# Decay attention, soft MoE and GELU layer on one core: the order of work in a pair of heads changed, one score product instead of two, and the first expert's w1 loaded last

## What is computed

```python
for t in range(S):                      # _attn_ref, r k v w: [4, 8, 768, 48]
    cur = einsum('bhd,bhe->bhde', u * kt, vt)
    y[:, :, t] = einsum('bhd,bhde->bhe', rt, state + cur)
    state = wt[..., None] * state + einsum('bhd,bhe->bhde', kt, vt)
logits = x @ phi                        # _moe_ref, x: [3072, 384]
d = softmax(logits, 0); slot_input = d.T @ x
slot_out[e] = relu(slot_input[e] @ w1[e]) @ w2[e]
x = softmax(logits, 1) @ slot_out
h = x @ w_in                            # _moe2_ref
out = (h * sigmoid(1.702 * h)) @ w_out
```

## Time and profile before

| what | value |
|---|---|
| profiled execution | 416.04 us |
| its span, first to last instruction | 414.1 us |
| TensorE busy | 400.3 us, 97% of the span |
| VectorE, ScalarE, GpSimd busy | 250.2, 186.8, 49.0 us |
| granted TensorE clock, mean | 1.000 |
| DMA | 69.00 MB, mean 167 GB/s |

### The profile page before, as it was taken

The page is one execution under the profiler, slowest core; times in us unless marked ns, Lnnn a source line. Parts: engine busy times, 40 slices in busy tenths (PEclk is TensorE's granted clock), DMA queues, the critical chain, the costliest instruction groups (busy, mean ns, idle before and its releaser), DMA issues.

```text
span 414.1 us, 9544 instructions
## 1 busy us (share of the span) xinstructions
PE 400.3 (97%) x3723; PEld 315.3 (76%) x3723; DVE 250.2 (60%) x463; ACT 186.8 (45%) x412; POOL 49.0 (12%) x50
## 2 busy tenths in 40 slices
PE   7989999999999879999999999999999999999996
PEld 5868787887888633545888888888888888888885
DVE  5878877987888574515767445454544545454542
ACT  5667777786787411504443422422242242224221
POOL 3432342233422200000000000000000000000000
PEclk9999999999999999999999999999999999999999
DMA  7999999899899398993000200010010001001001
GB/s 260 405 357 342 350 351 335 298 351 350 298 343 356 140 408 354 368 406 126 1 0 2 78 0 0 9 67 2 0 76 0 0 9 69 0 2 76 2 0 76
DMA packets 15589, 69.00 MB, mean 167 GB/s; under 512 B 1600, under 2 KB 1728, under 8 KB 14528
## 3 DMA queue, kind: packets, MB, share of 16 engines
q1 hardware_dynamic: 15552, 68.47, 44.0%
HBM read 63.75 MB, written 4.72 MB: 165 GB/s over the span
## 4 chain that ended last, share of the span: by engine, by line
PE 87%; DVE 5%; DMA 3%; ACT 3%; issue 2%; DVEq 0%; SPq 0%; ACTq 0%
PE bank L1022 31%; PE bank L1026 16%; PE bank L996 5%; PE bank L761 5%; PE bank L856 4%; PE bank L833 4%; PE bank L923 3%; PE bank L957 3%; PE bank L848 3%; DMA rk<-rk_in 2%; PE bank L767 2%; PE bank L799 2%; PE bank L814 2%; PE bank L790 2%; PE bank L774 1%
## 5 line engine op out<-in xcount | busy, mean ns | idle before, releaser
L522 ACT ACTIVATE ring<-bank 128x512 f32<-128x512 f32 x96 | 57.4, 598 | 139.4 <-PE bank L996 139.3
L728 DVE CAST g_hi<-ring 128x512 fp32r<-128x512 f32 x96 | 40.8, 425 | 88.8 <-ACT ring L522 88.8
L1022 PE MATMUL bank<-g_hi,wo_hi 128*128 128x512 f32 x285 | 80.1, 389 | 0.0
L1022 PE MATMUL bank<-g_hi,wo_lo 128*128 128x512 f32 x285 | 80.0, 389 | 0.0
L1026 PE MATMUL bank<-g_lo,wo_hi 128*128 128x512 f32 x285 | 80.0, 389 | 0.0
L730 DVE TENSOR_TENSOR g_lo<-ring,g_hi 128x512 fp32r<-128x512 f32 x96 | 66.5, 693 | 3.3
L1022 PEld LDWEIGHTS bank<-g_hi,wo_hi 128*128 128x128 f32 x285 | 53.4, 188 | 11.2 <-DVE g_hi L728 0.2
L1022 PEld LDWEIGHTS bank<-g_hi,wo_lo 128*128 128x128 f32 x285 | 53.5, 188 | 11.1
L1026 PEld LDWEIGHTS bank<-g_lo,wo_hi 128*128 128x128 f32 x285 | 53.5, 188 | 11.1
L996 PE MATMUL bank<-cst,mst 128*128 (+1 forms) x96 | 37.4, 391 | 0.1
L596 DVE TENSOR_TENSOR at<-bank,causal 128x512 f32<-128x512 f32 x48 | 30.1, 683 | 12.0 <-PE bank L833 11.7
(11 more groups left out here) (137 smaller groups left out, 440.7 us busy)
## 6 DMA issues: line engine op xcount, KB each, us to landing
nat<-nat_in SPq DMA_DIRECT2D x32, 576.0 KB, 6.0
rk<-rk_in SPq DMA_DIRECT2D x16, 768.0 KB, 7.0
ring<-w_in SPq DMA_DIRECT2D x16, 768.0 KB, 7.8
w2a<-w_in SPq DMA_DIRECT2D x4, 1536.0 KB, 12.4
out_t<-ring SPq DMA_DIRECT2D x5, 768.0 KB, 3.5
ring<-w_in SPq DMA_DIRECT2D x2, 1536.0 KB, 8.3
ring<-win_in SPq DMA_DIRECT2D x4, 768.0 KB, 10.2
ring<-wout_in SPq DMA_DIRECT2D x4, 768.0 KB, 15.0
```

The costliest lines, as they stand in the source:

```text
L522: a.activation(gact[:, s % NG, :], bank[6 + s % 2][:, :], ACT.Gelu_apprx_sigmoid).then_inc(g_done, 1)
L728: v.tensor_copy(g_hi[:, s % NG, :], gact[:, s % NG, :]).then_inc(ghi_done, 1)
L1022: t.matmul(bank[3 * par + o][:, :], wo[:, f, P * o:P * (o + 1)], g_hi[:, s % NG, :], start=(f == 0 and wo is wo_hi), stop=False)
```

## The change

- log_sums of the next pair stands whole (twelve records, one semaphore step) behind the scores; before, half of it stood ahead of them. exps waits for the whole, and makes both inverses first, then both exponentials.
- A score unit is one product of 128 keys against 128 tokens; the memsets of banks 2 to 4 go, with the wait for them.
- The x transposes of both halves stand together behind both halves of the value products; ScalarE evacuates both y halves first, then both x tiles.
- The logarithm is taken one pair ahead instead of two, ahead of scaled_states; w is rolled by one pair, and only w of pair 0 is loaded on its own.
- VectorE does the bonus of a pair ahead of front of the next pair. GpSimd's first product of each pair waits for front (f_done) of that pair.
- Both halves of w1 of expert 0 are loaded behind the loop instead of ahead of it.

```diff
@@ sync
-            sp.dma_start(w01[:, 0, :], w01_in[0]).then_inc(ld_w[0], 16)
+            sp.dma_start(w0, w0_in).then_inc(ld_w, 16)
             load_rk(0, 0)
-            sp.dma_start(w01[:, 1, :], w01_in[1]).then_inc(ld_w[1], 16)
...
-            load_w1(0, 0)
-            load_w1(0, 1)
             with sp.Fori(1, PAIRS // 2) as m:
...
+            for q in range(2):
+                load_w1(0, q)
             sp.dma_start(w2_early[:, :], w2_in[NE - 1]).then_inc(ld_w2[NE - 1], 16)
@@ gpsimd, pair
                 if s.first:
                     pool.wait_ge(ld_u, 16)
-                    pool.wait_ge(f_done, 1)
+                pool.wait_ge(f_done, s.i + 1)
@@ scalar
-                if not s.first:
-                    act.wait_ge(logsum_done, 2 * s.i)
+                    held = s.after(-1)
+                    w = nat[:, held.slot, 2, :]
+                    act.wait_ge(ld_wr[held.slot], 16 * held.loads + 16)
+                    act.wait_ge(logsum_done, s.i)
...
+                act.wait_ge(logsum_done, s.i + 1)
                 for q in range(2):
-                    act.wait_ge(logsum_done, 2 * s.i + q + 1)
                     a.activation(pinv[0:DP, G3 * q:G3 * (q + 1), :], src[q], ACT.Exp, scale=-1.0).then_inc(inv_done, 1)
+                for q in range(2):
                     a.activation(pw[0:DP, G3 * q:G3 * (q + 1), :], src[q], ACT.Exp).then_inc(exp_done, 1)
...
                 spread_decay(s)
+                if s.after(1) is not None:
+                    logs(s.after(1))
                 scaled_states(s)
...
-                if s.after(2) is not None:
-                    logs(s.after(2))
...
-                    if xg is not None and xg < G3:
+                if xg is not None and xg < G3:
+                    for q in range(2):
                         xt_evacuate(b, 2 * xg + q)
@@ vector
-            for q in range(2, 8):
+            for q in (5, 6, 7):
                 v.memset(bank[q][:, :], 0.0).then_inc(const_dve, 1)
...
-                n1 = s.after(1)
-                if n1 is not None:
-                    front(n1)
                 bonus(s)
+                if s.after(1) is not None:
+                    front(s.after(1))
@@ tensor
-                if n1 is not None:
-                    log_sums(n1, 0)
                 pe.wait_ge(rc_done, s.i + 1)
...
-                    for early in (MID, 0):
-                        ins = t.matmul(bank[2 + u // 4][early:early + MID, P * (u % 4) + early:P * (u % 4 + 1)],
-                                       k[rows, P * c + early:P * c + early + MID], r[rows, P * c + early:P * (c + 1)],
-                                       start=True, stop=True)
+                    ins = t.matmul(bank[2 + u // 4][:, P * (u % 4):P * (u % 4 + 1)],
+                                   k[rows, P * c:P * (c + 1)], r[rows, P * c:P * (c + 1)], start=True, stop=True)
...
                 if n1 is not None:
-                    log_sums(n1, 1)
+                    log_sums(n1)
...
-                    if xg is not None and xg < G3:
+                if xg is not None and xg < G3:
+                    for q in range(2):
                         x_transposes(b, 2 * xg + q)
```

More of the change, by code:

```diff
@@ L139, in decay_attention_soft_moe_gelu_kernel @@
         ld_rk = [sem(f"ld_rk{i}") for i in range(2)]
-        ld_w = [sem(f"ld_w{i}") for i in range(2)]
+        ld_w = sem("ld_w")
         ld_vk = [sem(f"ld_vk{i}") for i in range(2)]
@@ L396, in _, with logs @@
                 act.sem_inc(o_out[par], 1)
[L398 to L401, removed]
-                else:
-                    w = w01[:, early, :]
-                    act.wait_ge(ld_w[early], 16)
-                if not s.first:
-                    act.wait_ge(logsum_done, 2 * s.i)
+            def logs(s):
+                if s.first:
+                    w = w0
+                    act.wait_ge(ld_w, 16)
+                else:
+                    held = s.after(-1)
+                    w = nat[:, held.slot, 2, :]
+                    act.wait_ge(ld_wr[held.slot], 16 * held.loads + 16)
+                    act.wait_ge(logsum_done, s.i)
                 a.activation(lw.rearrange("p c (h e) -> p (c h) e", h=HP)[:, :, 0:D],
@@ L412, in exps @@
                     act.wait_ge(f_done, s.i)
+                act.wait_ge(logsum_done, s.i + 1)
+                src = [bank[q][0:DP, 0:G3 * (P + 1)].rearrange("p (c t) -> p c t", c=G3) for q in range(2)]
                 for q in range(2):
-                    act.wait_ge(logsum_done, 2 * s.i + q + 1)
-                    src = bank[q][0:DP, 0:G3 * (P + 1)].rearrange("p (c t) -> p c t", c=G3)
-                    a.activation(pinv[0:DP, G3 * q:G3 * (q + 1), :], src, ACT.Exp, scale=-1.0).then_inc(inv_done, 1)
-                    a.activation(pw[0:DP, G3 * q:G3 * (q + 1), :], src, ACT.Exp).then_inc(exp_done, 1)
+                    a.activation(pinv[0:DP, G3 * q:G3 * (q + 1), :], src[q], ACT.Exp, scale=-1.0).then_inc(inv_done, 1)
+                for q in range(2):
+                    a.activation(pw[0:DP, G3 * q:G3 * (q + 1), :], src[q], ACT.Exp).then_inc(exp_done, 1)
             def k_natural(s):
@@ L475, in _ @@
             act.wait_ge(const_dve, 1)
-            logs(FIRST, 0)
+            logs(FIRST)
             exps(FIRST)
-            logs(FIRST.after(1), 1)
             for k in range(-1, PPB - 1):
@@ L563, in _ @@
             v.memset(frep[:, :], 0.0).then_inc(const_dve, 1)
-            dve.wait_ge(const_dve, 9)
+            dve.wait_ge(const_dve, 6)
             for r in range(2):
@@ L756, in stay_warm, with log_sums @@
                     t.matmul(bank[to][:, 0:2 * P], ones_b[:, 0:P], ones_b[:, :], start=True, stop=True)
-            def log_sums(s, q):
+            def log_sums(s):
                 pe.wait_ge(ln_done, s.i + 1)
-                for c in range(G3 * q, G3 * (q + 1)):
-                    ins = t.matmul(bank[q][0:DP, (c % G3) * (P + 1):(c % G3 + 1) * (P + 1)], lw[:, c, 0:DP], tri[:, :],
+                for c in range(NC):
+                    ins = t.matmul(bank[c // G3][0:DP, (c % G3) * (P + 1):(c % G3 + 1) * (P + 1)], lw[:, c, 0:DP], tri[:, :],
                                    start=True, stop=True)
@@ L868, in _ @@
             pe.wait_ge(const_pool, 5)
-            for q in range(2):
-                log_sums(FIRST, q)
-            pe.wait_ge(const_dve, 9)
+            log_sums(FIRST)
             stay_warm(12, 3)
+            pe.wait_ge(const_dve, 4)
             pe.wait_ge(const_pool, 14)
@@ L1062 @@
         "rk_in": np.ascontiguousarray(np.stack([channels_first(r), channels_first(k)], axis=2)),
[L1063 to L1064 removed]
+        "w0_in": tokens_first(w)[0],
+        "nat_in": np.ascontiguousarray(np.stack([tokens_first(v), tokens_first(k), np.roll(tokens_first(w), -1, axis=0), tokens_first(r)], axis=2)),
         "u_in": u.reshape(1, H // 2, 2 * D),
```

6 lines of the change are left out of this document (2 added, 4 removed).

## The result

The changed kernel takes **410.79 us** (median of 4 runs, 410.70 to 410.89), the kernel before on the same chip 415.67 us (4 runs, 415.28 to 417.17). The ratio is 0.9876, 95% interval 0.9851 to 0.9901: faster by 1.2%, or 4.9 us. The profiled execution took 410.70 us with a span of 409.0 us, against 416.04 and 414.1.

The account below looks back on a forecast made before the run. TensorE, 97% busy, bounds the kernel, though pairs 1 to 4 wait for VectorE. Start +0.3, pairs 1–4 22.77 for 24.83, pairs 4–15 90.27 for 93.22: -4.7 from 415.52 gives 410.8 us, range 408.6 to 414.0.

Parts of the forecast that it names:

- log_sums together: TensorE, next pair's log_sums: one group of twelve takes 1.50 us instead of 1.69 in two groups, saving 0.19.
- One score product: TensorE, scores: two 64x64 products become one of 128 columns, 12 rounds still 1.47 us, plus 0.02 for a longer first load.
- the rival of the weights: TensorE, scores: 128 weight columns cannot load side by side, 1.3 us more per pair, 430 us; chance 0.05.
- x transposes together: TensorE, end of a pair: values and x transposes unbroken instead of 2.44 us in four pieces, saving 0.28.
- A pair with x transposes: Period between k transposes, TensorE the bound: 7.90 us instead of 8.25, or 9.23 where slot logits follow.
- The rival of another engine binding these pairs: VectorE's or ScalarE's chain 0.45 us longer than added up in pairs with x transposes: 413.8 us; chance 0.12.
- Pairs without: Pairs without x transposes, VectorE the bound: period 7.59 us instead of 8.28.
- Start: Pair 0: exps wait for all log_sums and the bonus joins the path, so pair 1's scores start 0.3 us later.
- the start pays more: Rival: pairs 1 to 4 run 0.3 us faster each and u lands a microsecond earlier, 408.9 us; chance 0.1.
- Logarithm one ahead: ScalarE: the logarithm before scaled_states fits where ScalarE waits for the scan anyway; cover 0.5 us in one late case, more elsewhere.
- Transfers: Rival: loads hold the loop at 341 GB/s, a period of 8.07 us, giving 414.2 us; chance 0.09.
- Bonus ahead of the next k: VectorE order: next k transposes can start 5.68 us after the scores; hidden with x transposes, otherwise period 7.59 for 8.28.

## Why the prediction was right, point by point

The forecast was 410.8 us and the median is 410.79. That they agree to 0.01 us is luck. The predicted gain was 4.7 us, the medians differ by 4.9 and the two profiles, at the scores of pair 15, by 5.1; the kernel before, against which the gain was set, was 0.15 us slower in these runs than the 415.52 of the prediction. The starts of the scores show where the rest lies. Changed kernel, pair 15:

```profile
131.62 1.61 PE L830 MATMUL bank<-rk 48*128 48x128 f32 x24
```

| stretch, start of scores | before | predicted | after |
|---|---|---|---|
| to pair 1 | 18.65 | 18.95 | 18.61 |
| pair 1 to 4 | 24.83 | 22.77 | 22.65 |
| pair 4 to 15 | 93.22 | 90.27 | 90.36 |
| pair 15 at | 136.70 | 132.0 | 131.62 |

- **log_sums together**: predicted 1.50, measured 1.51 (50.78 to 52.29). The switch from updates to scores, taken at 0.02 above 0.59, costs nothing: 0.58.
- **One score product**: 12 rounds take 1.54 us, not 2.8, so the rival of the weights did not occur. But the term was mis-sized: 0.02 for a longer first load, measured 0.07 (1.54 against 1.47), inside its bounds of 0 and 0.3. Over 15 spans this edit costs about 0.9 us (an estimate from 7.84 for 7.90 and 7.47 for 7.52), and the prediction did not have its other side, the stops, of which its one profile of the kernel before has none.
- **x transposes together**: 2.16 us predicted and measured. The 0.07 lost at k_natural is there: L799 to L814 is 1.40 us in one pair (47.26 to 48.66) and 1.41 in another, 1.33 in four, 1.27 before.
- **A pair with x transposes**: predicted 7.90, measured 7.88 to 7.98; with slot logits 9.23 and 9.25. (As written, the terms add up to 7.89 and 9.22, 0.1 us less over the nine. The rival of another engine binding these pairs did not occur; its losses as listed are 3.3 to 3.8 us, not 3.)
- **Pairs without**: predicted 7.59, measured 7.52 to 7.61. L799 waits 0.28 and 0.37 us for L578 there, as foretold.
- **Start**: predicted 0.3 us later, measured 0.04 earlier. The product that waits for u started at 11.17, not 11.35, and k transposes of pair 1 came at 16.73, not 17.0. What the prediction called a rival ("the start pays more") went a small part of its way.
- **The twelve log_sums of rows 4**, from which the 1.50 was taken, ran at full clock from the first one on, as the granted clock rose at 4.24 us there. In eight of the other thirteen profiles the row is 1.93 to 2.73 us, from which the term would have come out too large.
- **Logarithm one ahead**: no wait of L407 for a load. Taken back with the single w tile it costs 1.9 us, more than the 0.9 us or so that an earlier u explains.
- **Transfers**: no k multiply of the changed kernel waits for a load; its loop ran at 328 to 365 GB/s in windows of 10 and 15 us. For the shorter period of the experiments the traces show 388. The Trainium skill (SBUF — State Buffer, section "A bandwidth-pool intuition that's wrong") puts HBM to one core at about 358 GB/s; the 388 of the window above goes past that, so the measurement decides, and the 0.5 us it would have added in the prediction did not come.
- **w1 last**: the prediction needed rk of pair 2 to be early. With the bonus ahead of the multiply the load of 22.63 would do too, so no worth of this edit is shown (0.36 us in the medians, with overlapping ranges). In the kernel before, where k stood ahead of the bonus, the same load made VectorE wait 2.14 us; no run has both edits taken back.

What the prediction got wrong is not a number of the sum but **whom it thanks**. It put the whole gain of the pairs without x transposes on the order on VectorE, "Bonus ahead of the next k". Undone alone, that order is worth 0.65 us in all and nothing in the three spans from pair 1 to 4 (22.60 us for 22.65), since the wait only moves to the carried states. That the prediction's 7.59 held is right for its mechanism: with this order VectorE's chain does bind, at 5.72 us for 5.68. That the other order would have kept the 8.28 is what the runs deny. log_sums behind the scores is what it rests on: with the halves apart, the same VectorE order makes every span 8.36 (9.76 with slot logits) and the kernel slower than before. The prediction had the piece for this (1.91 us from k transposes to scores, which was 2.73 with half of log_sums inside) but used it inside a sum and did not price it as a condition. Taken back, the edits cost 1.1, 0.65, 0.36, 2.4, 1.9 and 7.4 us in the medians (the last on top of the 1.9; the first and third with ranges that overlap the changed kernel's), 13.8 in all, for a change that gained 4.9 to 5.1: they are not additive. The cycle gives the reason for the largest: it costs that much with VectorE's chain as the other half. What log_sums together would be worth on the kernel before was not run, nor were the new order of the exponentials and GpSimd's wait for front taken back.

What stays open: why some instruction packets are late with two products per score, and why the granted clock rises at 4.24 us in one execution and at 7.16 in another with the same products ahead of it.

## What to carry to other kernels

Price an order by start-to-start steps of the engine that is the bound, and then write the loop as one cycle: how long from A's start to B's on the one engine, how long from B's to the next A's on the other. A piece of work between the two that neither needs is paid in full, and moving it behind B can be worth more than merging it (here 0.85 us of the cycle against the 0.17 that the prediction had for the merging). Then undo the edits one at a time, as the sum tells the total but not who earned it.

An instruction count is a price of its own: a form that is 0.07 us shorter per pair by its records was 0.7 to 1.1 us slower in the median, with overlapping ranges.

Before two profiles are compared, look at where each granted clock rises: here it moved the start by up to 1 us, as much as some of the edits are worth, and made one edit that changes nothing in the spans look like a gain of 0.9 us.

## What the hardware showed that was not expected

- Stops of 0.20 to 0.93 us inside a group of products, only with two products per score, each ending 1.31 to 1.43 us after a packet of instructions has landed. The three kernels of that kind have spreads over their runs of 2.9 to 4.8 us; of the nine with one product, seven have 0.3 to 1.2, and two have one far run each (2.0 and 2.9 us), whose mean granted clock is 0.996 and 0.994.
- The granted clock rose between 4.24 and 7.16 us in fourteen profiles with the same warm-up products from 1.3 us on. The first twelve log_sums take 1.54 to 1.62 us where it rose by 4.82, and 2.40 to 2.73 where it rose at 6.49 or later.
- After 2 us in which TensorE was busy for 0.39, its granted clock fell to 0.51 and then 0.64 of full speed for 2 us each, and the execution was 1.6 us above its kernel's median.
- Loads into one core at 388 GB/s over 10 us while TensorE was busy for all of it.
